# Turning the hidden rows of a mixture-of-experts block: transposing DMAs in 16-bit halves in place of eight TensorE transposes

## The reference

```python
def _moe_ref(x, w_gate, w_noise, noise, w1, w2):      # x 2304 x 512, w1 8 x 512 x 1024, w2 8 x 1024 x 512
    ...                                               # noisy logits, top2, top2_w
    for e in range(E):
        for k in range(2):
            mask = top2[:, k] == e
            ...
            h = np.maximum(x[mask] @ w1[e], 0.0)
            out[mask] += top2_w[mask, k, None] * (h @ w2[e])
```

## Time and profile before

| | us |
|---|---|
| median of 3 runs | 1269.68 |
| the profiled execution's own time | 1269.59 |
| its span | 1267.9 |
| experts' stage, about | 266 to 801 |
| PE busy | 1235.0 |
| ACT busy | 490.2 |
| DVE busy | 493.5 |
| POOL busy | 367.6 |

### The profile page before, as it was taken

How to read it: one execution, slowest core, us unless ns; L and a number is a source line. 1 busy time by engine, 2 the same in 40 slices (tenths; PEclk the granted TensorE clock), 3 DMA queues, 4 the chain that set the end, 5 groups by cost and what they waited for, 6 DMA issues and landing times.

```text
span 1267.9 us, 23613 instructions
## 1 busy us (share of the span) xinstructions
PE 1235.0 (97%) x7378; PEld 1075.0 (85%) x7379; DVE 493.5 (39%) x900; ACT 490.2 (39%) x1068; POOL 367.6 (29%) x415
## 2 busy tenths in 40 slices
PE   8899999999999999999999999899999999999998
PEld 7677777788888888888888888799999999999997
DVE  7689998544050605141424070522131322213111
ACT  5688887533333334333343333312122121221211
POOL 4224443224453534454444473310010100100000
PEclk9899999989999999999999999999999999999999
DMA  4734342553243663424242411301010100100000
GB/s 102 200 85 102 88 94 52 175 177 85 78 137 99 215 206 109 129 86 145 70 149 78 137 50 34 108 18 59 1 51 25 50 25 0 50 25 0 25 1 25
DMA packets 102953, 106.06 MB, mean 84 GB/s; under 512 B 70666, under 2 KB 70816, under 8 KB 102876
## 3 DMA queue, kind: packets, MB, share of 16 engines
q1 hardware_dynamic: 85372, 68.56, 18.2%
q0 software_dynamic: 7280, 20.86, 6.1%
q10 hardware_dynamic: 10256, 16.06, 3.6%
HBM read 84.47 MB, written 22.81 MB: 85 GB/s over the span
## 4 chain that ended last, share of the span: by engine, by line
PE 86%; DVE 6%; issue 3%; DMA 1%; ACT 1%; SPq 1%; DVEq 0%; ACTq 0%; POOL 0%; POOLq 0%
PE PB L1721 10%; PE PB L1722 10%; PE PB L1720 10%; PE PD L1720 9%; PE PD L1722 9%; PE PD L1721 9%; PE PA L1722 4%; PE PA L1720 4%; PE PA L1721 4%; PE PC L1755 3%; PE PC L1551 3%; PE PA L1728 1%; PE PB L1609 1%; DVE Q L1147 1%; DVE probT L1157 1%
## 5 line engine op out<-in xcount | busy, mean ns | idle before, releaser
L1385 DVE CAST WX<-raw 128x1024 fp32r<-128x1024 f32 x56 | 54.2, 967 | 275.2 <-DMA raw<-in_moe_w 275.2
L829 POOL TENSOR_TENSOR hsTl<-hsT,hsTh 128x512 fp32r<-128x512 f32 x84 | 124.3, 1502 | 113.0 <-ACT hsT L1055 113.0
L1428 DVE TENSOR_TENSOR gv<-sig,PB 128x384 f32<-128x384 f32 x72 | 39.9, 555 | 298.8 <-PE PB L1722 298.7
L1720 PE MATMUL PB<-WX,xsTh 128*128 x344 | 138.1, 402 | 2.0 <-POOL xsTl L820 1.5
L1722 PE MATMUL PB<-WX,xsTl 128*128 x344 | 135.3, 393 | 0.0
L1721 PE MATMUL PB<-WX,xsTh 128*128 x344 | 135.3, 393 | 0.0
L1720 PE MATMUL PD<-WX,hsTh 128*128 x336 | 135.2, 402 | 0.0
L1722 PE MATMUL PD<-WX,hsTl 128*128 x336 | 131.6, 392 | 0.0
L1721 PE MATMUL PD<-WX,hsTh 128*128 x336 | 130.9, 390 | 0.0
L1093 ACT ACTIVATE sig<-PA 128x384 f32<-128x384 f32 x72 | 35.4, 492 | 186.9 <-PE PA L1722 186.9
L900 ACT ACTIVATE prob<-scores,nmax 128x128 f32<-128x128 f32 (+4 forms) x160 | 95.7, 599 | 25.8 <-DVE nmax L1178 24.3
(11 more groups left out here) (266 smaller groups left out, 2654.3 us busy)
## 6 DMA issues: line engine op xcount, KB each, us to landing
raw<-in_moe_w SPq DMA_DIRECT2D x28, 1024.0 KB, 5.2
y_d<-ys ACTq DMA_DIRECT2D x43, 256.0 KB, 2.7
out<-fin SPq DMA_DIRECT2D x18, 256.0 KB, 2.2
RT<-r_d SPq DMA_DIRECT2D x30, 144.0 KB, 3.0
qin<-in_q SPq DMA_DIRECT2D x32, 128.0 KB, 2.4
vin<-in_v SPq DMA_DIRECT2D x32, 128.0 KB, 2.4
raw<-in_moe_w ACTq DMA_DIRECT2D x4, 1024.0 KB, 10.0
x_d<-xtok SPq DMA_DIRECT2D x8, 512.0 KB, 3.3
```

Of the source, the lines that this page charges most:

```text
L829: nc.gpsimd.tensor_tensor(hsTl[:, cols], hsT[:, cols], hsTh[:, cols].bitcast(F32), ALU.subtract).then_inc(hTl_done, 1)
L1385: nc.vector.tensor_copy(high, source).then_inc(w_high, 1)
L1428: nc.vector.tensor_tensor(gv[:, :], sig[:, :], PB[:, 512 * (f % 2):512 * (f % 2) + GN], ALU.mult).then_inc(gv_done, 1)
L1720: pe.matmul(acc, hi, w_hi, start=first, stop=False)
```

## The change

- TensorE's eight transposes of a block go, in 42 of 43 blocks; the last block keeps the old way. The loop is hidden(i), in(i+1), out(i-1).
- `block_hidden` makes its product half by half (512 columns each), and says after each half that it is there (`h_made` counts 2 a block).
- `halves_split`: ScalarE copies a half out of PSUM as two planes of 16-bit numbers, the upper and lower halves of each float32: 128 x 1024 16-bit values in `halves_in`.
- `halves_turn`: ScalarE issues one transposing DMA a half, eight 128 x 128 squares of 16-bit values, from `halves_in` to `halves_T`, of which there is one for both halves.
- `join`: GpSimd puts the 16-bit planes together as float32 in `hsT`.
- `hidden_relu` and `hidden_high`: ScalarE applies the rectifier in place on `hsT`, then copies it as high part to `hsTh`. GpSimd makes the low part as before.
- `halves_in` and `hsT` of one half lie in the same place, so a split waits for the low part of the block before; `hs` is used by the last block alone. `table` moves to another place in SBUF.

ScalarE's loop body before. `[waits ...]` names the semaphores; ISA and REGISTER_ALU rows are bookkeeping.

The diff, without the tile declarations and the last block's part:

```diff
+            def join(i, n):
+                pool.wait_ge(h_turned, 16 * (PARTS * i + n + 1))
+                nc.gpsimd.tensor_copy(hsT[n][:, :].bitcast(U16).rearrange("p (f x) -> p x f", x=2), halves_T[:, :, :]
+                                      ).then_inc(h_joined, 1)
...
+            def hidden_low(i, n):
+                pool.wait_ge(hT_copied, PARTS * i + n + 1)
...
+            def block(i, more=True):
+                join(i, 0)
+                rows_low(i + 1)
+                if more:
+                    gather(i + 2)
+                join(i, 1)
+                for n in range(PARTS):
+                    hidden_low(i, n)
...
+            def halves_split(i, n):
+                act.wait_ge(h_made, PARTS * i + n + 1)
+                at_least(act, hTl_done, PARTS * i + n - 1)
+                nc.scalar.activation(halves_in[n][:, :, :],
+                                     PB[:, F // PARTS * n:F // PARTS * (n + 1)].bitcast(U16)
+                                     .rearrange("p (f x) -> p x f", x=2), ACT.Copy).then_inc(h_copied, 1)
+            def halves_turn(i, n):
+                act.wait_ge(h_copied, PARTS * i + n + 1)
+                at_least(act, h_joined, PARTS * i + n)
+                act.dma_start(halves_T[:, :, :].rearrange("p x (c t) -> p (x c) t", t=P),
+                              halves_in[n][:, :, :].rearrange("p x f -> p (x f)"), transpose=True).then_inc(h_turned, 16)
+            def hidden_relu(i, n):
+                act.wait_ge(h_joined, PARTS * i + n + 1)
+                nc.scalar.activation(hsT[n][:, :], hsT[n][:, :], ACT.Relu).then_inc(h_relu, 1)
+            def hidden_high(i, n):
+                act.wait_ge(h_relu, PARTS * i + n + 1)
+                nc.scalar.activation(hsTh[:, F // PARTS * n:F // PARTS * (n + 1)], hsT[n][:, :], ACT.Copy
+                                     ).then_inc(hT_copied, 1)
...
+            def block(i):
+                halves_split(i, 0)
+                halves_turn(i, 0)
+                halves_split(i, 1)
+                block_in(i + 1)
+                halves_turn(i, 1)
+                hidden_relu(i, 0)
+                if not isinstance(i, int):
+                    block_out(i - 1)
+                hidden_high(i, 0)
+                hidden_relu(i, 1)
+                hidden_high(i, 1)
...
-                for c_ in range(DC):
-                    for z in range(2):
+                for z in range(2):
+                    at_least(pe, h_copied, PARTS * i + z - 1)
+                    for c_ in range(DC):
                         last = three(PB[:, 512 * z:512 * z + 512], xsTh[:, P * c_:P * c_ + P],
...
-                last.then_inc(h_made, 1)
+                    last.then_inc(h_made, 1)
...
             with pe.Fori(1, BLOCKS - 1) as i_:
                 block_hidden(i_)
                 block_in(i_ + 1)
                 block_out(i_ - 1)
-                block_turned(i_)
```

More of the change, by code:

```diff
@@ L27 @@
 U32 = mybir.dt.uint32
+U16 = mybir.dt.uint16
 ALU = mybir.AluOpType
@@ L125, in __call__ @@
             n *= x
-        n *= size or (2 if dt in (BF16, F16) else 4)
+        n *= size or (2 if dt in (BF16, F16, U16) else 4)
         t = self.nc.alloc_sbuf_tensor_at(name, shape, dt, offset=self.at)
@@ L257, in program @@
         xsTl = g("xsTl", [P, DM], F32R)
+        hidden_at = g.at
         hs = g("hs", [P, F], F32)
         hsTh = g("hsTh", [P, F], F32R)
-        hidden_low_at = g.at
         hsTl = g("hsTl", [P, F], F32R)
         ys = g("ys", [P, DM], F32)
+        halves_at = g.at
+        halves_T = g("halves_T", [P, 2, F // PARTS], U16)
         assert g.at <= end, (g.at, end)
         xsT = Places(nc, rows_low_at)("xsT", [P, DM], F32)
-        hsT = Places(nc, hidden_low_at)("hsT", [P, F], F32)
+        h16 = Places(nc, hidden_at)
+        halves_in = [h16(f"halves_in{n}", [P, 2, F // PARTS], U16) for n in range(PARTS)]
+        h32 = Places(nc, hidden_at)
+        hsT = [h32(f"hsT{n}", [P, F // PARTS], F32) for n in range(PARTS)]
         n_ = Places(nc, free_at)
@@ L308, in program @@
         x2l.append(y("x2l1", [P, DC, GN], F32R))
-        gv = Places(nc, g.at)("gv", [P, GN], F32)
-        assert max(y.at, g.at + 4 * GN) <= end, (y.at, g.at, end)
+        gv = Places(nc, halves_at)("gv", [P, GN], F32)
+        assert y.at <= halves_at and halves_at + 4 * GN <= end, (y.at, halves_at, end)
         def turning(g, i):
@@ L821, in rows_low @@
                                         ).then_inc(xsl_done, 1)
-            def hidden_low(i):
-                for n in range(PARTS):
-                    cols = slice(F // PARTS * n, F // PARTS * (n + 1))
-                    pool.wait_ge(hT_copied, 2 * PARTS * i + 2 * n + 2)
-                    pool.sem_inc(pool_passed, 1)
-                    nc.gpsimd.tensor_tensor(hsTl[:, cols], hsT[:, cols], hsTh[:, cols].bitcast(F32), ALU.subtract
-                                            ).then_inc(hTl_done, 1)
+            def join(i, n):
+                pool.wait_ge(h_turned, 16 * (PARTS * i + n + 1))
+                pool.sem_inc(pool_passed, 1)
+                nc.gpsimd.tensor_copy(hsT[n][:, :].bitcast(U16).rearrange("p (f x) -> p x f", x=2), halves_T[:, :, :]
+                                      ).then_inc(h_joined, 1)
+            def hidden_low(i, n):
+                cols = slice(F // PARTS * n, F // PARTS * (n + 1))
+                pool.wait_ge(hT_copied, PARTS * i + n + 1)
+                pool.sem_inc(pool_passed, 1)
+                nc.gpsimd.tensor_tensor(hsTl[:, cols], hsT[n][:, :], hsTh[:, cols].bitcast(F32), ALU.subtract
+                                        ).then_inc(hTl_done, 1)
+            def block(i, more=True):
[4 more added lines that the diff above has]
+                join(i, 1)
+                for n in range(PARTS):
+                    hidden_low(i, n)
             gather(0)
             gather(1)
-            rows_low(1)
-            gather(2)
-            hidden_low(0)
+            block(0)
             with pool.Fori(1, BLOCKS - 2) as i_:
-                rows_low(i_ + 1)
-                gather(i_ + 2)
-                hidden_low(i_)
-            rows_low(BLOCKS - 1)
-            hidden_low(BLOCKS - 2)
+                block(i_)
+            block(BLOCKS - 2, more=False)
             pool.wait_ge(tab_loaded, 16)
@@ L1048, in last_turned @@
                     nc.scalar.activation(hsTh_z[:, cols], PC[:, cols], ACT.Copy).then_inc(hT_copied, 1)
-            def block_turned(i):
-                act.wait_ge(h_turned, i + 1)
-                for n in range(PARTS):
-                    cols = slice(F // PARTS * n, F // PARTS * (n + 1))
-                    nc.scalar.activation(hsTh[:, cols], PC[:, cols], ACT.Copy).then_inc(hT_copied, 1)
-                    nc.scalar.activation(hsT[:, cols], PC[:, cols], ACT.Copy).then_inc(hT_copied, 1)
             def block_out(i):
@@ L1063, in block_out @@
                 act.dma_start(y_d.rearrange("(i p) n -> i p n", p=P)[i], ys[:, :]).then_inc(y_stored, 16)
+            def block(i):
[10 more added lines that the diff above has]
+                hidden_high(i, 1)
             block_in(0)
-            block_hidden(0)
-            block_in(1)
-            block_turned(0)
+            block(0)
             nc.scalar.activation(warm[:, :], ident[:, 0:1], ACT.Sigmoid)
@@ L1071, in _ @@
             with act.Fori(1, BLOCKS - 1) as i_:
-                block_hidden(i_)
-                block_in(i_ + 1)
-                block_out(i_ - 1)
-                block_turned(i_)
-            block_hidden(BLOCKS - 1)
+                block(i_)
+            last_hidden()
             last_turned()
@@ L1786, in _ @@
                 block_out(i_ - 1)
-                block_turned(i_)
             block_hidden(BLOCKS - 1)
-            block_out(BLOCKS - 2, between=lambda: block_turned(BLOCKS - 1))
+            block_out(BLOCKS - 2, between=last_turned)
             block_out(BLOCKS - 1, rows=(hsTh_z, hsTl_z))
```

24 lines of the change are left out of this document (14 added, 10 removed).

## The result

The changed kernel took 1318.74 us (median of 4 runs, 1314.13 to 1321.31) beside 1269.92 us for the kernel before on the same chips: a ratio of 1.0389 (95% interval 1.0361 to 1.0417), 49 us slower. The forecast was slower, 1333 us, range 1240 to 1530.

What follows compares the result with a forecast made beforehand. TensorE's own work was taken to set the 12.30 us turn. From 1269.6 us: 33 quiet turns -12, loads +54, splits +20, start about +1, together +63, giving 1333 us; range 1240 to 1530.

Steps and rivals of the forecast that it cites:

- What goes: TensorE in the experts' stage: removed transposes save 0.87 us a turn, 12.30 to 11.43; 36.5 us possible gain in all.
- The second loop: Split, two transposing DMAs, joins and low part around the one halves_T: 5.34 us + 2D a turn, bounding above D = 3.05.
- D: Time from a transposing DMA's issue to its landing: 3.3 us in quiet stretches, 6.5 us while weights arrive.
- signs of being wrong: Joins of 2 us or more, an issue holding ScalarE over 0.5 us, or landing times unchanged beside loads.
- The rule that transposing DMAs are as fast as regular ones: Skill's rule for transposing DMAs: D would be 2.3 us in quiet stretches and the sum near 1240 us.
- Beside loads: Nine turns in the experts' stage during weight loads: D 6.5 us, turn 18.3, 6.0 more than before; +54 us.
- second effect: Next rows' low part waits behind the first join; TensorE's next block_hidden starts about 3.9 + D after the split; not added.
- Beside splits: GpSimd's three loop operations slow by 0.74 us each beside VectorE's weight splits: +2.2 us a turn, about 9 turns, +20 us.
- Quiet turns: 33 turns of the experts' stage without disturbance: 11.94 us each, 0.36 less than before; -12 us.
- As quick as an ordinary DMA: Rival: D 2.3 us, 3.5 beside loads, mostly hidden behind TensorE; 1234 to 1250 us, middle 1243; chance 0.26.
- One square after another: Rival: the DMA's eight squares go serially, D 14.4 us, turn 34.1; about 2190 us, or down to 1600; chance 0.07.
- The clock's lower level: TensorE after waits: granted clock may fall to 1.2 GHz, up to 1.6 us a turn in the slow-DMA case; nothing added.

Runs made afterwards that it cites:

- 3: Changed kernel with a halves_T and semaphore for each half, so the second transposing DMA no longer waits for the first join: 1317.63 us, ratio 1.0382.
- 6: Two-buffer kernel with the 16-bit copies (halves_in) in a place of their own, so the next split no longer waits for GpSimd's low part: 1319.72 us, ratio 1.0390.
- 10: Kernel with two buffers, copies apart, low part of the rows and gather before the joins; ScalarE does both joins instead of GpSimd: 1266.23 us, ratio 0.9984.
- 11: Kernel before the change with only its first product made half by half: 1269.03 us, ratio 1.0002.
- 2: Changed kernel with weight loads from expert 2 on cut to 8 columns a chunk, VectorE still splitting whole chunks: 1296.38 us, ratio 1.0214.
- 1: Changed kernel without weight loads and weight splits of experts 2 to 7; the gated layer's loads stay: 1279.63 us, ratio 1.0068.
- 9: Kernel with 16-bit copies apart and the rows' low part first; GpSimd also issues the gather before both joins: 1317.96 us, ratio 1.0388.
- 7: Kernel with 16-bit copies apart; GpSimd makes the low part of the next block's rows before the first join: 1308.79 us, ratio 1.0334.
- 4: Two-buffer kernel with GpSimd's gather of the block after next moved behind the second join: 1365.45 us, ratio 1.0762.

## Why the prediction was right, step by step

**What goes.** TensorE's own turn was put at 11.43 us; it is 11.36 where nothing else binds (experiments 3, 6, 10). The order of the product was given no cost, and has none (11).

**The second loop.** 5.34 us + 2D was the sum. With D = 3.1 it gives 11.54; the nine shortest turns are 11.54 to 11.77, most of them 11.63 to 11.70. The join was too small (1.07 taken, 1.34 found) and some hops too large (0.18 taken from the end of the first join to the issue, 0.09 found). The prediction closed the loop by the low part on GpSimd and had the two copies on ScalarE beside it; they end within 0.11 us of each other (610.57 and 610.68), and the split starts at 610.60. D in quiet stretches was taken as 3.3 and is 3.1. The issue took 1.26 us where the ordinary one has 0.34 in the earlier trace rows. This was one of the prediction's signs of being wrong (above 0.5), but it did not put ScalarE's copies on the loop: in the turn shown they were done at 603.57, and the second issue waited for the join until 604.69.

The rule that transposing DMAs are as fast as regular ones (the Trainium skill, "Advanced Engine Details and Errata", X-Bar Transpose (TRN2)) does not hold for the landing time here: 3.1 us beside 2.3 for the store in the earlier trace rows. That store goes to HBM and the transposing DMA from SBUF to SBUF; an ordinary DMA of this size within SBUF was not run. The 1309 ns for one square (the Trainium skill, "VectorE: DVE Perf Modes", The three transpose paths) do not multiply: eight squares land in 3.1 us.

**Beside loads.** The place was right; the size and the path were not. I had both transposing DMAs of nine turns at 6.5 us, +54 us, of which the experts' loads (24 x 5.3 us, seven turns) are 42. Measured, one DMA of each expert's load is late, at 5.9 to 6.3 us. These six were issued between 0.13 us ahead of a 1 MB load and 0.51 us behind its start, and landed 0.9 to 1.0 us after it; six others, issued 3.2 us into such a load, landed after 3.1 us all the same. The surplus landing time is 37.8 us over the whole stage, and leaving out the experts' loads gave back 22.4 us (experiment 2; the other layers' loads stayed).

Nor was it the loop over the one `halves_T` that cost the time there. The prediction named a second effect, TensorE's next product behind the low part of its rows and the first join, and did not add it because it "decides later than the first loop". TensorE's waits are just that: 36.7 us in 21 turns for `xsTl`, and 4.4 us in 5 for `hsTl`. With a buffer for each half and with the 16-bit copies apart these waits stayed, at 38.1 and 42.8 us (experiments 3 and 6).

**Beside splits.** +20 us forecast, 16.8 measured (experiments 1 and 2). The join's mean is 1.48 us over all turns, 2.8 at most.

**Quiet turns.** 33 turns were to gain 0.36 us each. Only 9 turns come out short, and gain 0.64 (one of them beside splits); the rest lie beside loads or splits or recover from a long turn, and stay near 12.2 to 13.4. The sum, +63 us, stands against 49.

**Luck in the sum.** It is nearer than its parts. The experts' loads were put 20 us too high (42 against 22.4) and the splits 3 us. What is left of the forecast when both are taken off is 63 - 42 - 20 = +1 us, and experiment 1 shows 9.7: too low by 9. The direction and the disturbed turns were foreseen; that the total came within 14 us is in part two errors against each other.

**The rivals.** "As quick as an ordinary DMA" was too low on D (2.3 against 3.1, and 3.5 against 6.0 beside loads) and wrong on the outcome: in experiment 1, where the disturbance is smallest, the change still gains nothing. "One square after another" fell with the first landing time. The clock's lower level was given no cost, because TensorE would have more slack than that. It had none in the long turn shown, and some 15 us of the loss, by the estimate above, are matmuls at 0.43 us. What I did not see ahead: that the order and the two joins of GpSimd's list matter more than the single `halves_T`. The prediction named the buffer as the thing to blame. In quiet turns it was (11.65 to 11.36 us with a second one), but over the whole program giving each half its own changed nothing (3), and cutting the loop altogether changed nothing (6). Taking the joins off GpSimd, in a kernel that had both of these already, gave back the whole loss (9 to 10).

## What to carry to other kernels

Here a step taken off the engine that bounds was paid with latency elsewhere: write down the loop that closes over its buffers, and count every operation that stands in an in-order list between two links of it, not only the links. A loop with no slack in quiet turns loses in each disturbed one, so look at what runs beside it (here weight loads and VectorE's splits). Count what a wait costs the bounding engine behind it too (here the lower clock). And where removing one wait brings another of the same length, as it did in experiments 6, 7 and 9, try moving work off the engine that all of them wait for.

## What the runs showed of the hardware

- A DMA that transposes 128 x 1024 16-bit values from SBUF to SBUF landed after 3.1 to 3.2 us in 69 of 84 cases, against 2.3 us for an ordinary 256 KB store to HBM, and its issue held ScalarE's queue for 1.26 us: the copy behind it started 1.56 us after the one before it ended.
- Issued 0.07 us behind a 1 MB load, it landed about 1 us after that load; issued 3.24 us behind one, it landed after 3.1 us as without a load. With a second transposing DMA issued 2.1 to 2.7 us into the load, the longest landing was 10.3 and 14.2 us, and the loads beside them took 9.7 and 13.4 (experiments 3 and 4; the longest 1 MB load of this stage took 8.4 us in the kernel before).
- The ordinary DMAs beside it slowed too: the store of `ys` from a median of 2.7 to 3.8 us, the gather of `xs` from 3.4 to 4.2 in the loop.
- GpSimd and VectorE were slower beside each other: the 54 joins with no VectorE work beside them took at most 1.36 us, the other 30 took 1.72 at the mean and up to 2.83, and VectorE's subtraction of a chunk, 1.53 us at the mean before, took 1.99 after.
- After a wait of 2.32 us TensorE's granted clock was 0.60 of full speed over 4 us, and seven matmuls stood 0.43 us apart instead of 0.23.
- The same copy of 1024 16-bit elements took ScalarE 1.02 us from PSUM into planes and 1.37 us from SBUF back into pairs.
